# One program for the recurrence and the gated layer, with weights and first input prepared inside the recurrence's last chunks, and attention's first input loaded in the layer before it

## The reference

```python
# 1. recurrence: r, k, v, w are [4, 8 heads, 768, 48], u is [8, 48]
for t in range(S):
    cur = einsum('bhd,bhe->bhde', u * k[t], v[t])
    y[t] = einsum('bhd,bhde->bhe', r[t], state + cur)
    state = w[t][:, :, :, None] * state + einsum('bhd,bhe->bhde', k[t], v[t])
x = y.transpose(0, 2, 1, 3).reshape(B, S, 384)
# 2. gated layer: w_in [384, 1024], conv_w [3, 1024], w_out [1024, 384]
h = maximum(x @ w_in, 0)
c = conv_w[0] * h[s-1] + conv_w[1] * h[s] + conv_w[2] * h[s+1]
z = (h * sigmoid(c)) @ w_out
# 3. attention with 4 experts of width 64, the two best of each token weighted by a gate
for e in range(4):
    q, k, v = z @ wq[e], z @ wk[e], z @ wv[e]
    a = softmax(causal(q @ k.T / 8))
    out += gate_weight(z @ w_gate, e) * (a @ v @ wo[e])
```

## Time and profile before

| what | us |
|---|---|
| median of three executions | 671.43 (671.18 to 677.67) |
| the profiled execution | 671.61 |
| its span, first to last instruction | 669.9 |
| recurrence, until PE's last matmul of it ends | 150.6 |
| gated layer, first matmul of a product to the last | 163.5 to 381.8 |
| attention, first projection to the end | 394.9 to 669.9 |
| PE busy over the whole span | 598.4 (89%) |

### The profile page before, as it was taken

One profiled execution on the slowest core, in us unless ns is written; L12 is line 12 of the kernel. 1 busy time (PEld: TensorE's weight loads), 2 busy tenths in 40 slices (PEclk: granted clock), 3 DMA queues, 4 the chain that ended last, 5 costly groups with the idle time before them and its releaser, 6 DMA issues. The chain is left out here.

```text
span 669.9 us, 11883 instructions
## 1 busy us (share of the span) xinstructions
PE 598.4 (89%) x4505; PEld 492.7 (74%) x4505; DVE 425.5 (64%) x747; ACT 352.2 (53%) x812; POOL 130.3 (19%) x142
## 2 busy tenths in 40 slices
PE   1899989992799999999999649799999999999886
PEld 0777767772799999999999549576677767676545
DVE  6799999944556666666666342655764665456653
ACT  2557656755556656655665332544643454343540
POOL 1444444401000000000000010422232133132330
PEclk9989989996899999999999859899999999999999
DMA  8459899417200030040010050200000210001001
GB/s 346 147 104 207 173 327 199 134 38 190 82 0 1 37 105 1 1 141 0 0 71 1 0 212 1 70 1 1 27 23 13 83 37 13 13 13 48 13 12 71
DMA packets 22263, 49.55 MB, mean 74 GB/s; under 512 B 6924, under 2 KB 14500, under 8 KB 21348
## 3 DMA queue, kind: packets, MB, share of 16 engines
q1 hardware_dynamic: 22212, 48.85, 24.8%
HBM read 34.69 MB, written 14.16 MB: 73 GB/s over the span
## 5 line engine op out<-in xcount | busy, mean ns | idle before, releaser
L1042 POOL TENSOR_SCALAR att_a<-att_a,att_rden,att_gate 128x128 f32<-128x128 f32 (+5 forms) x96 | 68.4, 722 | 191.8 <-DVE att_rden L1181 191.8
L1173 DVE TENSOR_REDUCE att_nmax<-att_ps 128x1 f32<-128x128 f32 (+5 forms) x96 | 55.2, 617 | 52.3 <-PE att_ps L1290 52.3
L73 PE MATMUL hid_ps<-hid_g_lo,hid_w_hi 128*128 128x384 f32 x192 | 67.2, 350 | 6.3 <-DVE hid_g_lo L803 6.2
L73 PE MATMUL hid_ps<-hid_x_lo,hid_w_hi 128*128 128x384 f32 x192 | 66.4, 346 | 6.2 <-ACT hid_conv_sb L766 5.4
L793 DVE SCALAR_TENSOR_TENSOR hid_cv<-hid_h,hid_conv_sb,hid_cv 128x768 f32<-128x768 f32 x64 | 65.0, 1016 | 2.4 <-ACT hid_cv L726 1.2
L75 PE MATMUL hid_ps<-hid_g_hi,hid_w_hi 128*128 128x384 f32 x192 | 66.0, 344 | 0.0
L74 PE MATMUL hid_ps<-hid_g_hi,hid_w_lo 128*128 128x384 f32 x192 | 66.0, 344 | 0.0
L74 PE MATMUL hid_ps<-hid_x_hi,hid_w_lo 128*128 128x384 f32 x192 | 65.8, 343 | 0.0
L75 PE MATMUL hid_ps<-hid_x_hi,hid_w_hi 128*128 128x384 f32 x192 | 65.7, 342 | 0.0
L1071 ACT ACTIVATE att_a<-att_ps,att_nmax 128x128 f32<-128x128 f32 (+5 forms) x96 | 59.9, 633 | 3.9 <-DVE att_nmax L1173 3.6
L1081 ACT ACTIVATE att_at<-att_ps 128x512 f32<-128x512 f32 (+2 forms) x64 | 27.1, 449 | 63.9 <-PE att_ps L1315 63.6
(11 more groups left out here) (145 smaller groups left out, 1326.6 us busy)
## 6 DMA issues: line engine op xcount, KB each, us to landing
rec_kr<-in_kr_img SPq DMA_DIRECT2D x10, 576.0 KB, 10.0
rec_kr<-in_kr_img SPq DMA_DIRECT2D x3, 1536.0 KB, 9.2
rec_v_n<-in_v_img SPq DMA_DIRECT2D x8, 576.0 KB, 10.9
x_features<-rec_x_p SPq DMA_DIRECT2D x16, 288.0 KB, 10.4
hid_x_t<-x_features SPq DMA_DIRECT2D x12, 384.0 KB, 5.3
z_features<-hid_z_t SPq DMA_DIRECT2D x4, 1152.0 KB, 4.8
att_z_t<-z_features SPq DMA_DIRECT2D x12, 384.0 KB, 4.3
out_y<-att_o_sb SPq DMA_DIRECT2D x24, 192.0 KB, 1.9
```

What stands on the lines that cost most here:

```text
L73: nc.tensor.matmul(dst, xh, yl, start=start, stop=False, skip_group_check=True)
L1042: G.tensor_scalar(probs, probs, rden[:, t:t + 1], gate[:, b % 2, 2 * ep + odd, i:i + 1], ALU.mult, ALU.mult).then_inc(a_scaled, 1)
L1173: V.tensor_reduce(nmax[:, t:t + 1], ps[:, lo:lo + n], AX_X, ALU.max, negate=True).then_inc(nmax_ready, 1)
```

## The change

`recurrence` and `hidden` become one function, `features`, with one block. The instructions of both stay, with these differences:

- The convolution weights are loaded at the start (`load_conv`, fourth DMA of SP), and turned and copied behind the first `gather`. `scores(1)` waits for that copy, because it uses the same bank.
- ACT splits the layer's weights in six pieces of 1024 columns, one behind `take_y` of each chunk 12 to 17. DVE does the rest part of the first three at chunks 19 and 20. POOL does the rest part of the other three, in a loop that stands behind its last products of the recurrence.
- x of batch 0 is loaded while the recurrence still runs (behind the store of half batch 5), into the third slot of k and r. ACT splits it behind `take_y` of chunks 20 and 21, DVE at chunks 21 and 22.
- PE does `make_h(0, 0)` ahead of the last `output`, and `make_h(0, 1)` behind it.
- The loops over batches are written out. x and the attention weights are loaded behind the last store of x. Several buffers of the layer lie in buffers that the recurrence has done with: `shared` (k and r, later x, a convolution buffer and the attention weights), `spare` (the recurrence's `x_p`) and the raw weights.
- z of batch 0 is loaded from HBM into `spare` in the layer's last batch, so attention finds it on chip.
- In attention the first four projections of batch 0 are one plain float32 matmul for each three before, straight from the raw weights and raw z; they wait only for the weights' loads. The order of the splits is turned: z first, then the weights of v and the output, then those of q and k.

```diff
+            for n in range(FT, NW):          # POOL, behind its loop over half batches
+                split_w(n)
...
+                if N - C - NW <= i < N - C:  # ACT, at the end of chunk i
+                    split_w(i - (N - C - NW))
+                if N - 4 <= i < N - 2:
+                    split_x(0, i - (N - 4))
...
+                if i == N - 5:               # DVE, at the end of chunk i
+                    split_w(0)
+                if i == N - 4:
+                    split_w(1)
+                    split_w(2)
+                if N - 3 <= i < N - 1:
+                    split_x(0, i - (N - 3))
...
+            turn_conv()                      # PE
             for i in range(N):
                 if i + 1 < N:
                     scores(i + 1)
...
+                if i == N - 1:
+                    make_h(0, 0)
                 output(i)
...
+            make_h(0, 1)
...
+                if b == B - 2:               # SP, in the layer's loop over batches
+                    sp.wait_ge(z_stored, 16 * (b + 1))
+                    sp.dma_start(spare[:, 0:FT * S].rearrange("p (t s) -> p t s", t=FT),
+                                 z_dram[0].rearrange("(t p) s -> p t s", p=P)).then_inc(z_first, 16)
...
+                    if b == 0 and n < 4:     # PE, project_z
+                        m = mm(dst[:, 0:HALF], (whole_wq if what == "q" else whole_wk)[:, t, 0:P],
+                               first_z[:, t, HALF * where[1]:HALF * (where[1] + 1)], start=(t == 0), stop=(t == FT - 1),
+                               skip_group_check=True)
...
-            pe.wait_ge(c_ready, 4)
+            pe.wait_ge(weights.loaded, weights.N_LOADED)
             for n in range(NPJ):
                 project_z(0, n)
+            pe.wait_ge(c_ready, 4)
```

More of the change, by code:

```diff
@@ L152, in recurrence @@
     LEAD = 2
-    TOP = 64 + D
+    FT = F // P
+    FF = weights.raw_in.shape[2]
+    NF = FF // P
+    HALF = S // 2
+    NZ = 2 * FT
+    LAG = 2
     with ExitStack() as ctx:
@@ new lines, in split_x, with rectify @@
+            def split_x(b, half):
+                if b == 0:
+                    act.wait_ge(bont_psum, NB)
+                else:
+                    wait(act, h_psum, 2 * NF * b - 1 + half)
+                if half == 0:
+                    act.wait_ge(s_x, 16 * (b + 1))
+                tokens = slice(HALF * half, HALF * (half + 1))
+                for t in range(FT):
+                    A.activation(x_hi[:, t, tokens], x_t[:, t, tokens], ACT.Copy).then_inc(x_hi_ready, 1)
+            def rectify(b, f):
+                wait(act, gated, NF * b + f - 1)
+                for half in range(2):
+                    act.wait_ge(h_psum, 2 * (NF * b + f) + half + 1)
+                    A.activation(h[:, f % 2, 1 + HALF * half:1 + HALF * (half + 1)],
+                                 bank[NZ + half][:, 0:HALF], ACT.Relu).then_inc(h_ready, 1)
+                act.wait_ge(h_ready, 2 * (NF * b + f) + 2)
+                A.activation(cv[f % 2], h[:, f % 2, 1:S + 1], ACT.Copy,
+                             scale=conv_sb[:, NF + f % NF:NF + f % NF + 1]).then_inc(cv1, 1)
@@ L365, in _ @@
             take_ks(0)
+            act.wait_ge(conv_psum, 1)
+            A.activation(conv_sb[:], bank[3][:, 0:3 * NF], ACT.Copy).then_inc(conv_ready, 1)
             own(1)
@@ L464, in mask, with prepare @@
+            def prepare(hb, stage):
+                if stage == 0:
+                    products(hb)
+                    scan(hb)
+                elif stage == 1:
+                    invert(hb)
+                    between_chunks(hb)
+                else:
+                    for part in range(3):
+                        decay(hb, part)
             def mask(i):
@@ new lines, in add_z @@
+            def add_z(b, f):
+                if b == 0 and f == 0:
+                    pe.wait_ge(out_split, FT)
+                    pe.wait_ge(a_ready, 2 * N)
+                    pe.wait_ge(y_taken, N)
+                pe.wait_ge(g_split, NF * b + f + 1)
+                for n in range(NZ):
+                    cols, tokens = slice(P * (n // 2), P * (n // 2 + 1)), slice(HALF * (n % 2), HALF * (n % 2 + 1))
+                    if f == 0:
+                        wait(pe, z_taken, NZ * (b - 1) + n + 1)
+                    m = product(nc, bank[n][:, 0:HALF], (out_hi[:, f, cols], out_lo[:, f, cols]),
+                                (g_hi[:, f % 2, tokens], g_rest[:, f % 2, tokens]), f == 0, f == NF - 1)
+                m.then_inc(g_used, 1)
@@ L863, in batch, with attention @@
+            make_h(0, 1)
+            for b in range(B):
+                for f in range(NF):
+                    if f + LAG < NF or b + 1 < B:
                         make_h(b, f + LAG)
                     add_z(b, f)
-            pe.wait_ge(w_split, 1)
-            make_h(0, 0)
-            make_h(0, 1)
-            pe.wait_ge(w_split, 2)
-            each_batch_last(pe, B, batch)
-def attention(nc, z_dram, weights, out):
+def attention(nc, spare, z_dram, weights, out):
     B, F, S = z_dram.shape
@@ L937, in attention @@
         wo_parts = [weights.out_part(x) for x in (w_hi, w_lo)]
+        whole_wq, whole_wk = (weights.part(w_raw, start, E * HD) for start in (weights.WQ, weights.WK))
+        first_z = spare[:, 0:FT * S].rearrange("p (t s) -> p t s", t=FT)
         z_t = sb("z_t", [P, FT, S])
```

590 lines of the change are left out of this document (270 added, 320 removed).

## The result

The changed kernel took 666.11 us (median of 17 runs, 664.38 to 672.39), the kernel before 676.39 (17 runs, 671.18 to 689.18). The ratio is **0.9874, 95% interval 0.9845 to 0.9903**: 1.3% faster, about 8.5 us of the kernel before (the two medians are 10.3 apart). The three runs of before that stood ahead of the prediction had a median of 671.43, 5 us under that of all 17. So the forecast of 665.6 us was met to 0.5 us, but that closeness is in part luck: the change that it implied (665.6 / 671.43 = 0.9913) was too small by 2.6 us. The measured change lies beyond the 1% that the prediction took as the least that can be told, and the interval ends just short of it, at 0.97%; faster and same had stood at 47 and 48 in 100. The profiled executions differ by 6.34 us: 671.61 against 665.27, spans 669.9 and 663.6.

What follows compares the result with a forecast made beforehand. PE bounds the gated layer and the recurrence's last chunks, DVE the recurrence before them. Terms -14.0 + 1.2 + 6.9 + 2.3 + 0 - 2.2 = -5.8 took the profiled 671.61 to 665.8, as median 665.6 us; range 656 to 670.

Steps and rivals of the forecast that it cites:

- First hand-over, -14.0: From recurrence to gated layer: `add_z(0, 0)` would start at 164.9 in place of 178.87, 14.0 us earlier, nothing else disturbed.
- Convolution weights, +1.2: At the recurrence's front: turning and copying them ahead of `scores(1)` delays chunk 1, +1.2 us (0.5 to 2.3), not made up.
- POOL's pieces, +6.9: In half batch 7: three POOL pieces take turns with DVE's `decay` products, holding them 3 x 2.3 us (0 to 8.7).
- Half clock behind it, +2.3: Behind PE's wait for the held state scaling: about 5 us at half clock costs 2.3 us (1.4 to 3.2).
- The wait of 7.8 us that was to show it: PE's wait ahead of the `gather` of chunk 20, 0.91 us before, was to grow to near 8 us.
- ACT's pieces, 0: In the recurrence's later chunks: ACT's weight pieces of 1.0 us fit its idle time, cost 0 (to 1).
- Attention's start, -2.2: At attention's block: PE begins at once with float32 products, v at 401.6 in place of 403.82, -2.2 us (-4 to +4).
- A: Rival on half batch 7: POOL's pieces hold nobody, so no 6.9 and 2.3, giving 656.4 us; 20%.
- its half form: Only two of POOL's three pieces meet DVE's `decay`, giving 662.8 us; 10%.
- B: Rival on the last twelve chunks: ACT becomes the chain, its pieces delay in full, +9.0 us, giving 674.6; 5%.
- C: Rival on attention's start: clock stays low through 24 instructions, v at 407.7, +3.9 in place of -2.2, giving 671.7; 7%.

Runs made afterwards that it cites:

- Experiment 3: Changed kernel with POOL's three weight pieces given to DVE behind its pieces of x: 656.62 us, ratio to the kernel before 0.9683.
- experiment 4: Changed kernel with the convolution weights turned and copied in the last chunk, not behind chunk 0: 665.98 us, ratio to the kernel before 0.9810.
- experiment 5: Changed kernel with the output weights loaded behind the k and r image of half batch 6: 667.17 us, ratio to the kernel before 0.9881.
- experiment 1: Kernel before plus three unread POOL differences of 1024 columns behind its last half batch: 689.48 us against 680.47 beside it, ratio 1.0132.
- experiment 8: Changed kernel with attention's first input loaded in attention's own block, float32 projections kept: 671.63 us, ratio to the kernel before 0.9969.
- experiment 2: Changed kernel with POOL's three weight pieces waiting until DVE's decay of half batch 7 is done: 658.39 us, ratio to the kernel before 0.9691.
- 11: Changed kernel with POOL's pieces given to DVE, convolution weights turned in the last chunk, output weights loaded later: 656.64 us, ratio to the kernel before 0.9705.
- 12: Changed kernel with DVE making POOL's pieces, later convolution turning and output-weight load, early Sigmoid table, sigmoid(0,0) before the second Relu half: 651.11 us, ratio 0.9635.
- experiment 9: The changed kernel once more, unaltered: 667.91 us, ratio to the kernel before 0.9892.
- experiment 6: Changed kernel with each of ACT's six weight roundings made twice: 667.35 us, ratio to the kernel before 0.9884.
- experiment 7: Changed kernel with attention's first four projections as split products again, input still on chip: 669.90 us, ratio to the kernel before 0.9922.
- 10: Changed kernel with attention's first input loaded in its own block and its first four projections split again: 671.78 us, ratio to the kernel before 0.9943.

## Why the prediction was right, and where it was not

*First hand-over, -14.0.* Right. Built as 16.4 us from the start of `make_h(0, 0)` to `add_z(0, 0)`, it measured 16.65, with the wait of 3.48 us at its end (3.5 forecast). Experiment 3 gives it without the lock: 167.73 less 2.59 (the shift ahead of `decay`) is 165.14; forecast 164.9. One row was misread on the way, without effect: of the five waits of DVE for PE's scores in the earlier trace rows, three lie in chunks 20 to 22 (137 to 147 us) and not ahead of chunk 19.

*Convolution weights, +1.2.* Right in size at the front: from half batch 2 (47.68 before, 48.78 after, DVE's second product of `decay`) to half batch 5 (96.89, 97.99) all stands 1.1 us later, and experiment 4 takes 1.2 away. By half batch 7 it was 1.8 in the two profiled executions: 0.7 more came from something that the prediction had no term for. The output weights' load, which both kernels issue there, made the image of half batch 6 land later with the change than before it (experiment 5). But this stretch varies by more than that: from the scaling at about 101 us to the one ahead of `decay` it is 26.97 us in the kernel before and 27.64 in the changed one, 28.66 in its second profile, 30.07 in experiment 1 and 32.10 in experiment 8, and 26.41 to 26.44 in the three with the later load. Behind PE's wait of 1.9 us at 95 the half clock lasted 7 us in the first two and 16 or more in experiments 1 and 8, and there DVE waited for PE. In no time of experiments 4 and 5 does either piece show.

*POOL's pieces, +6.9.* Right: 6.45 in the changed kernel, 6.48 alone in the kernel before. Three products are held, each by 2.15 us where 2.3 were reckoned, whatever passes between two instructions included. The two ends of the range, 0 and 8.7, are both excluded for this kernel. In nine profiled executions with the pieces right behind POOL's last product, it took 12.86 to 12.90 us from scaling to scaling in eight and 10.93 in one (experiment 8); in the kernel before and the four without them there (2, 3, 11 and 12) it took 6.40 to 6.42. By the Trainium skill, SBUF — State Buffer, section Who interferes with whom, a VectorE instruction with two SBUF inputs and a GpSimd instruction that reads SBUF contend for one pair of ports, and whoever has it locks the other out. The trace agrees: 2.15 us for each of the three.

*Half clock behind it, +2.3.* Right for the profiled execution: 10.8 us (148.48 to 159.28) less the shift of 1.8 and the hold of 6.45 leaves 2.6. But it is no constant: 7.2 in the one profiled of experiment 4 (13.64 less 6.47). So the lock's whole price is 6.5 plus 2.6 to 7, and taking it away gave 9.5 by the medians. It may be part of why the changed kernel's runs spread over 8 us and the four of experiment 3 over 2.4, but it can't be all of it: the kernel before has no such wait and spreads over 18.

*The wait of 7.8 us that was to show it.* 4.22 in the profiled execution, 7.38 in experiment 9. The wait was reckoned against a PE at full clock one chunk earlier; after a wait of 1.92 us PE did that chunk at half clock and filled part of it. A wait is a difference of two engines' times, and worse evidence than DVE's own rows.

*ACT's pieces, 0.* Right, as far as can be told: with twice as many no cost is shown (experiment 6).

*Attention's start, -2.2.* The mechanism was right, **the size of the term was off**: v came 9.7 us behind the block's start and not 12.4. The step that failed is the price of a float32 matmul of 384 columns. The prediction had 0.42 us at full clock and 0.77 at half, with 0.1 for weights worked out from two matmuls of 192 columns. In the trace the first seven take 4.46 us at clock 0.51, 0.64 each, and the last 16 take the 5.2 us from 391.1 on at clock 1.00, 0.32 each (one stands across the change): the weights cost nothing, they load beside the matmul before. The 0.1 us had come from two matmuls of 192 columns (144.23 to 144.75), whose rows do not show what the rest of their time was. The Trainium skill, FP8 and Floating Point Precision, section TensorE Precision Notes, has four passes for a product; 4 x 384 columns at 2.4 GHz make 0.64 us for the two instructions of one product, an estimate, and the trace agrees to the hundredth (0.32 each). By that rule the prediction had v 10.2 us behind the block's start (399.4 less 389.2), which was the better number for this term. The half clock lasted 4.5 us, as reckoned (5). The two parts are worth 3.2 (experiment 7) and 3.8 us (8) to the start of v, 5.0 together (10): less than their sum, since either leaves PE waiting.

*The end.* Of the 4.93 us won there 1.2 were given back inside attention, where the mean clock of the last 93 us is 0.98 and was 1.00. The terms as measured make -2.56 to the block, -4.93 to v and +1.2: -6.3 for the forecast -5.8. The sum is close because errors offset each other: the block came 1.0 us later than forecast (-3.6), the start of attention gave 2.7 more, and 1.2 went again. As all executions together show some 8.5 us, the one profiled of before (671.61, median 676.39) was a fast one.

*The rivals.* A is excluded by 1 and, for the changed kernel as profiled, its half form too, though that form does occur (8); B is excluded by 6, C by v at 396.33 and by 10. The case for A was not idle as a design, though: its 656.4 is near what experiment 3 reaches when POOL's pieces really hold nobody (656.62), if also with some luck, as it started from the same 671.4 and the same -2.2.

## What to carry to other kernels

Work moved to an idle engine isn't free if it reads and writes the memory that the critical engine works from: ask for each DVE product with two operands in SBUF (the on-chip memory that is not PSUM) whether a POOL instruction can be running, and put POOL's long ones where DVE reads PSUM or is idle, or give them to DVE there. A wait of PE of some microseconds costs more than itself, by an amount that differs from run to run, so an edit that removes 1 us ahead of such a wait may show nothing, and the same edit pays once the wait is gone. Judge the parts of a change by rows at fixed marks (scaling, first product, block start) as well as by the time.

## What the runs showed of the hardware

- The half clock behind a wait of PE had different lengths for the same work: behind the lock's wait 5.7 us (experiments 1 and 9), 6.3 (the changed kernel), 7.7 (5), 15.6 (7) and 15.7 (4), behind `add_z(0, 0)` 2.7, 3.1 and 6.2, and in the middle of the recurrence 7 us in one execution of the kernel before and 16 in the same instructions of experiment 1. Ahead of chunk 19 it followed waits of 1.92 us (in the changed kernel and in experiments 2, 4, 5 and 7) and of 1.52 (6), and did not follow those of 0.61 and 1.20 us in the same place (9 and 3). What decides its length these runs do not show.
- DVE's `COPY_PREDICATED` with one operand in PSUM kept its 1.34 us while POOL's products ran beside it; only its products with both operands in SBUF were held (2.16 us for 1.20 in experiment 2, 3.10 for 0.95 in the changed kernel).
- Weights of 128x128 float32 loaded wholly beside the previous float32 matmul: of 24 instructions with a new weight each, those at full clock followed each other at 0.32 us, the time of two passes of 384 columns, and those at half clock at 0.64.
